# A fused attention, MLP and expert kernel: three blocks of the leading expert instead of two before the slot table

## What is computed

```python
# attention: B, H, S, D = 4, 8, 768, 48
for t in range(S):
    cur = np.einsum('bhd,bhe->bhde', u[None] * kt, vt)
    y[:, :, t] = np.einsum('bhd,bhde->bhe', rt, state + cur)
    state = wt[:, :, :, None] * state + np.einsum('bhd,bhe->bhde', kt, vt)
# MLP on x = y as [3072, 384]; w_in [384, 2048], w_out [2048, 384]
h = x @ w_in
g = np.maximum(h, 0.0) + alpha * np.minimum(h, 0.0)
x = g @ w_out
# top-1 of 8 experts; w1 [8, 384, 1024], w2 [8, 1024, 384]
logits = x @ w_gate
expert_idx = np.argmax(logits, axis=1)
...
for e in range(E):
    mask = expert_idx == e
    ye = np.maximum(x[mask] @ w1[e], 0.0) @ w2[e]
    out[mask] = gate_w[mask, None] * ye
```

## Time and profile before

| | |
|---|---|
| median of 3 runs | 789.07 us (788.85 to 791.1) |
| the profiled execution | 791.64 us, span 789.8 us |
| PE busy | 737.8 us, 93% |
| DVE, ACT, POOL busy | 469.9, 364.5, 391.7 us (59, 46, 50%) |
| mean granted PE clock | 0.979 |
| DMA | 171.61 MB, mean 217 GB/s |
| chain that ended last | PE 66%, DMA 8%, DVE 7%, POOL 5%, issue 5% |

### The profile page before, as it was taken

One profiled execution on the slowest core, in us unless ns is written; L12 is line 12 of the kernel. 1 busy time (PEld: TensorE's weight loads), 2 busy tenths in 40 slices (PEclk: granted clock), 3 DMA queues, 4 the chain that ended last, 5 costly groups with the idle time before them and its releaser, 6 DMA issues.

```text
span 789.8 us, 17773 instructions
## 1 busy us (share of the span) xinstructions
PE 737.8 (93%) x6779; PEld 518.4 (66%) x6779; DVE 469.9 (59%) x959; ACT 364.5 (46%) x734; POOL 391.7 (50%) x372
## 2 busy tenths in 40 slices
PE   4689989989999989999989999997999999999995
PEld 3447655656765666665666666656787878878783
DVE  7995877677768777786786763464433333333331
ACT  3652576647646756646756664462121221212210
POOL 6452567769759759778768875352010101101011
PEclk9987999999999999999999999998999999999998
DMA  8838318372653653645545245797799776776763
GB/s 345 330 131 236 134 62 298 110 250 92 220 213 119 231 211 121 230 140 193 193 151 180 80 160 191 285 419 271 259 394 381 282 246 223 239 263 214 251 232 115
DMA packets 42838, 171.61 MB, mean 217 GB/s; under 512 B 5214, under 2 KB 13152, under 8 KB 37120
## 3 DMA queue, kind: packets, MB, share of 16 engines
q1 hardware_dynamic: 30160, 108.18, 38.8%
q10 hardware_dynamic: 9072, 52.09, 18.7%
q0 software_dynamic: 3520, 10.17, 3.3%
HBM read 133.87 MB, written 37.33 MB: 217 GB/s over the span
## 4 chain that ended last, share of the span: by engine, by line
PE 66%; DMA 8%; DVE 7%; POOL 5%; issue 5%; ACT 3%; SPq 1%; ACTq 1%; POOLq 0%; DVEq 0%
PE bank L1687 5%; PE bank L1689 5%; PE bank L1688 5%; PE bank L1675 5%; PE bank L1676 5%; PE bank L1678 5%; PE bank L1833 4%; PE bank L1831 4%; PE bank L1832 4%; PE bank L1796 4%; PE bank L1797 4%; PE bank L1798 4%; DMA arena<-w_exp_dram 4%; PE bank L1647 2%; DMA route_rows<-xrow,pos 2%
## 5 line engine op out<-in xcount | busy, mean ns | idle before, releaser
L594 POOL TENSOR_TENSOR act_buf<-act_buf 128x384 f16<-128x384 f32 x128 | 119.6, 934 | 148.7 <-ACT act_buf L793 147.8
L1267 DVE SCALAR_TENSOR_TENSOR act_buf<-neg,slope,bank 128x384 f32<-128x384 f32 x128 | 77.8, 608 | 89.4 <-ACT neg L786 88.9
L1687 PE MATMUL bank<-arena,act_buf 128*128 128x392 f16 x384 | 128.2, 334 | 1.5 <-POOL act_buf L594 1.0
L682 POOL DMA_INDIRECT out_dram<-neg,dest x28 | 27.6, 984 | 203.0 <-DVE neg L1520 195.4
L1689 PE MATMUL bank<-arena,act_buf 128*128 128x392 f16 x384 | 128.1, 334 | 0.0
L1688 PE MATMUL bank<-arena,act_buf 128*128 128x392 f16 x384 | 128.1, 334 | 0.0
L1675 PE MATMUL bank<-xh,arena 128*128 128x384 f16 x384 | 126.8, 331 | 1.3 <-DVE act_buf L1267 0.6
L1676 PE MATMUL bank<-xl,arena 128*128 128x384 f16 x384 | 126.7, 331 | 0.0
L1796 PE MATMUL bank<-shared,arena 128*128 128x128 f16 x672 | 116.5, 221 | 1.4 <-DMA arena<-expert_split 1.4
L1797 PE MATMUL bank<-shared,arena 128*128 128x128 f16 x672 | 116.5, 221 | 0.0
L1798 PE MATMUL bank<-shared,arena 128*128 128x128 f16 x672 | 116.4, 221 | 0.0
(11 more groups left out here) (174 smaller groups left out, 1552.3 us busy)
## 6 DMA issues: line engine op xcount, KB each, us to landing
arena<-expert_split ACTq DMA_DIRECT2D x29, 1536.0 KB, 8.2
arena<-w_exp_dram SPq DMA_DIRECT2D x32, 768.0 KB, 7.5
expert_split<-arena SPq DMA_DIRECT2D x32, 768.0 KB, 5.4
arena<-expert_split SPq DMA_DIRECT2D x9, 1536.0 KB, 10.4
arena<-rk_in_dram SPq DMA_DIRECT2D x24, 512.0 KB, 5.5
arena<-rk_tok_dram SPq DMA_DIRECT2D x24, 384.0 KB, 3.6
arena<-w_dram SPq DMA_DIRECT2D x24, 256.0 KB, 6.4
shared<-route_rows ACTq DMA_DIRECT2D x31, 197.0 KB, 2.7
```

The source lines that it names most:

```text
L594: pool.tensor_tensor(gl[:, f % 4, :], gf[:, f % 4, :], gh[:, f % 4, :], ALU.subtract).then_inc(gl_done, 1)
L1687: pe.matmul(at, gh[:, f % 4, ts], woh[:, f, :], start=(f == 0), stop=False)
```

## The change

1. `EARLY = 3`: the leading expert does three blocks ahead of the table. All three use the resident leader weights in `w1_sb[0]` and `w1_sb[1]`. The third need not be full when it is chosen. Its row start is found by a short chain of six DVE steps from the final count (`third_*`), and `third_row_ready` lets ACT load it as soon as all scatters have landed, without the table. The PE order becomes `first(0)`, `first(1)`, `second(0)`, `second(1)` with `turn(2)` inside, `first(2)`, `turn(3)`, `second(2)`, and only then the wait for the table and `step(3)`.
2. The table takes three blocks off the leading expert, at least one is left (`ALU.max` with 1), so there can be one more slot (`SLOTS = 32`).
3. The slots behind take their first weights to `w1_sb[(n - 1) % 3]`; SP's load of expert 0's to `w1_sb[2]` waits for the third block's rows (`x_in[2]`).
4. The second weights of expert 0 are loaded behind half 2's pieces, of expert 1 ahead of half 7's, of experts 2 and 3 between them. Each has a semaphore of its own.
5. Units 50 and 51 get their low parts in half 6 (POOL), the last high of that half moves from f = 14 to 13, and the units of half 7 come at f = 0, 1, 3 to 12 instead of 2 to 13.
6. `load_early_rows` goes from f = 9 to 3, `load_early_w1` from 13 to 12, and `load_early_w2` from behind the last `hidden_high` to f = 15, ahead of `x_high(0)`.

```diff
-SLOTS = TOK // 128 + NE - 1
+SLOTS = TOK // 128 + NE
-EARLY = 2
+EARLY = 3
...
-        HI_AT, HI_AT_START, HI_AT_END = [0, 4, 6, 8, 9, 10, 12, 14], [11, 12, 13, 14], list(range(2, 14))
-        LO_AT, LO_AT_START, LO_AT_END = [4, 5, 7, 8, 9, 10], [12, 13, 14, 15], list(range(2, 14))
+        HI_AT, HI_AT_START, HI_AT_END = [0, 4, 6, 8, 9, 10, 12, 14], [11, 12, 13, 14], [0, 1] + list(range(3, 13))
+        LO_AT, LO_AT_START, LO_AT_END = [4, 5, 7, 8, 9, 10], [12, 13, 14, 15], [0, 1] + list(range(3, 13))
+        HI_AT_SEVENTH, LO_AT_SEVENTH = [0, 4, 6, 8, 9, 10, 12, 13], [4, 5, 7, 8, 9, 10, 13, 14]
...
             for g in range(1, 2 * B - 1):
                 middle(g, FIRST_UNIT[g] // 2)
-            load_w2(0)
+                if g == 2:
+                    sp.wait_ge(wide_free[0], 4)
+                    load_w2(0)
             sp.wait_ge(khat_done, 6 * B)
             sp.wait_ge(qt_done, 6 * B)
             sp.wait_ge(vl_done, 6 * B)
             sp.wait_ge(y_evac, UP + 6 * B)
+            load_w2(1)
             for j in range(FIRST_UNIT[2 * B - 1] // 2, 4 * NE - 1):
                 store_hu(j - 1)
                 load_hu(j + 1)
-                if j % 2 == 0:
-                    load_w2(1 + (j - FIRST_UNIT[2 * B - 1] // 2) // 2)
+                if j in (4 * NE - 5, 4 * NE - 3):
+                    load_w2(2 + (j - (4 * NE - 5)) // 2)
...
-            sp.wait_ge(w1_in[1], 16)
+            sp.wait_ge(x_in[2], 16)
             sp.dma_start(w1_sb[2], wsplit[0][:, 0:2 * UNIT]).then_inc(w1_in[2], 16)
...
-                        if end and f == 9:
+                        if end and f == 3:
                             load_early_rows()
-                        if end and f == 13:
+                        if end and f == 12:
                             load_early_w1()
                         if end and f == 15:
+                            load_early_w2()
                             x_high(0)
...
             hidden_high(2 * B - 1, NF - 1, True)
-            load_early_w2()
             x_high(1)
...
-            for n in range(EARLY):
+            for n in range(2):
                 h_high(n)
-            act.wait_ge(row_tab_ready, 1)
+            act.wait_ge(third_row_ready, 1)
             act.wait_ge(scattered, UPD + 16 * NC * 2 * B)
...
-            for n in range(EARLY, EARLY + 3):
-                load_x(n)
+            load_x(2)
+            act.wait_ge(row_tab_ready, 1)
+            load_x(3)
+            load_x(4)
+            x_high(2)
+            load_x(5)
+            h_high(2)
             act.wait_ge(tab_ready, 1)
-            load_w1(EARLY + 1)
-            x_high(EARLY)
+            load_w1(4)
+            x_high(3)
...
             h_low_part(0, 0)
             dve.wait_ge(rank_evac, 2 * B)
+            dve.scalar_tensor_tensor(out=third_sel[:, :], in0=pick_two[:, :], scalar=1.0 / EARLY, in1=next_row[:, 0:NE],
+                                     op0=ALU.mult, op1=ALU.mult).then_inc(third_chain, 1)
+            dve.wait_ge(third_chain, 1)
+            dve.tensor_reduce(third_row[:, :], third_sel[:, :], AX_X, ALU.add).then_inc(third_chain, 1)
...
+            dve.tensor_copy(slot_tab[0:1, 8:9], third_row[0:1, :]).then_inc(third_row_ready, 1)
...
             h_low_part(1, 1)
             y_out(0)
-            x_low(EARLY)
+            x_low(2)
+            y_out(1)
+            h_low(2)
+            x_low(3)
+            y_out(2)
...
-            for n in range(EARLY):
-                first(n, False)
-            for n in range(EARLY):
-                second(n, None)
+            first(0, False)
+            first(1, False)
+            second(0, None)
+            second(1, None)
+            first(2, False)
+            turn(3)
+            second(2, None)
+            pe.wait_ge(tab_ready, 1)
             for n in range(EARLY, MIN_RUN):
                 step(n)
```

More of the change, by code:

```diff
@@ L313, in build @@
         w1_in = [sem(f"w1_in{i}") for i in range(3)]
-        w2_in = sem("w2_in")
+        w2_in = [sem(f"w2_in{i}") for i in range(NE)]
         x_in = [sem(f"x_in{i}") for i in range(4)]
@@ L475, in middle @@
                     load_tok(b, half, 2)
-            for g in range(1, 2 * B - 1):
-                middle(g, FIRST_UNIT[g] // 2)
             def load_w2(e):
@@ L482, in load_w2 @@
                     sp.wait_ge(split_out[i], UP + 16 * (2 * e + 2))
-                if e > 0:
-                    sp.wait_ge(w2_in, 16 * e)
                 sp.dma_start(arena[:, w2_at(e):w2_at(e) + 2 * UNIT], wsplit[e][:, 2 * UNIT:4 * UNIT]
-                             ).then_inc(w2_in, 16)
-            load_w2(0)
+                             ).then_inc(w2_in[e], 16)
+            for g in range(1, 2 * B - 1):
+                middle(g, FIRST_UNIT[g] // 2)
+                if g == 2:
+                    sp.wait_ge(wide_free[0], 4)
+                    load_w2(0)
             sp.wait_ge(khat_done, 6 * B)
@@ L501, in _ @@
                 sp.wait_ge(split_out[i], UP + 32 * NE)
-            sp.wait_ge(w1_in[1], 16)
+            sp.wait_ge(x_in[2], 16)
             sp.dma_start(w1_sb[2], wsplit[0][:, 0:2 * UNIT]).then_inc(w1_in[2], 16)
-            for i in (2, 3):
-                sp.wait_ge(x_in[i], 16)
+            sp.wait_ge(x_in[3], 16)
             sp.wait_ge(w1_in[0], 32)
@@ L508, in _ @@
             for e in range(4, NE):
+                if e > 4:
+                    sp.wait_ge(w2_in[e - 1], 16)
                 load_w2(e)
@@ L620, in body @@
                         hidden_low(g, f)
-                        if g >= 2 and f == 0:
+                        if g >= 2 and not end and f == 0:
                             unit_low(unit - 2)
-                        if end and f == 1:
-                            unit_low(unit - 1)
                         if start:
@@ L873, in body @@
                     start, end = first and half == 0, last and half == 1
-                    highs = HI_AT_END if end else HI_AT_START if start else HI_AT
+                    highs = HI_AT_END if end else HI_AT_START if start else HI_AT_SEVENTH if g == SEVENTH else HI_AT
                     nb, nh = b + half, 1 - half
@@ L1821, in second @@
                 for f in range(NFE):
-                    if n == EARLY - 1 and f == NFE // 2:
-                        pe.wait_ge(tab_ready, 1)
-                        turn(EARLY)
+                    if n == 1 and f == NFE // 2:
+                        turn(2)
                     fs = slice(f * 128, (f + 1) * 128)
```

47 lines of the change are left out of this document (31 added, 16 removed).

## The result

| | before | after |
|---|---|---|
| median, 20 runs each | 789.14 us (784.65 to 794.83) | 785.54 us (780.0 to 791.83) |
| ratio of the runs | 1 | 0.9945, 95% interval 0.9926 to 0.9964 |
| the profiled execution | 791.64 us | 784.04 us, span 782.3 us |
| PE busy | 737.8 us | 733.9 us |
| mean granted clock | 0.979 | 0.986 |

The kernel became faster by 0.55%: 3.6 us between the medians, 4.3 by the ratio. The profiled executions are 7.6 us apart, more than the change is worth. Half 0, whose code is the same, took 74.97 us in one and 72.09 in the other, since PE's clock fell behind two waits in the first trace (0.50 and 0.66 in the 5 us behind 54.7 and 104.6) and behind the first of them alone in the second (0.66 behind 52.9, 1.00 behind 101.5).

A forecast was written before the change was run, and what follows sets the result against it. PE is busy 93%, so only its waits and slow clock can be won. Of 9.17 us at the change of phase 4.0 return; plus 1.56 in half 7, less 0.4 and 0.6: 5.7 us, giving 783.4 us, range 781.5 to 788.0.

The forecast's parts named there:

- before `second(2)`: Third block: `second(2)` follows `first(2)` with only a turn between, so PE waits 1.1 us for ACT and DVE.
- ACT's place at f = 15: End of half 7: second weights' load ahead of `x_high(0)` in ACT's queue loses 0 to 1.5 us, taken as 0.4.
- After half 7: At `rank(7)`: a wait of 1.08 us instead of 0.71 and 3.77, with no slow clock following.
- DVE becomes late: Middle of `first(1)`: PE waits a new 1.82 us for the low split of (0, 1), behind part of the slot table.
- The last store: End of half 7: last store of splits issued at about 526.7 instead of 533.17, landing 6 to 9.08 us later.
- Second weights of expert 0: Half 3: the 1.5 MB load just before a scatter costs PE between nothing and 3.0 us, taken as 0.6.
- Splits earlier: Halves 6 and 7: two low splits move to half 6, and both waits of half 7 go, 1.56 us won.
- Slots 3 and 4: Weights of slots 3 and 4: no wait, or 4 us at worst for slot 4; the old 1.00 goes.
- Third block: From `first(1)` to `first(3)`: rows arrive in time, so the 1.16 us before `turn(2)` goes; 1.1 comes before `second(2)`.
- A: Change of phase: clock falls all the same behind the waits of 1.08 and 1.82; 785.9 us at worst; chance 0.10.
- B: DMA moves: half 3's scatter costs 3.0 us, or `turn(2)` still waits 1.8, or both (787.6 us); chance 0.22.
- C: ACT's new place for the second weights: if the last store lands late, 1.3 us slower, 790.4 us; chance 0.05.

The follow-up runs named there:

- again: The changed kernel unaltered, profiled and timed a second time beside its variants: 787.28 us, ratio 0.9967 to the kernel before.
- e7: Kernel before with only the phase 1 moves (points 4 to 6), two early blocks and the old slot table: 785.69 us, ratio 0.9943.
- e9: Kernel before with only the new tables of splits, all loads at their old places and two early blocks: 789.31 us, ratio 0.9984.
- e10: Phase 1 moves with two early blocks, but expert 0's second weights mid half 3 and `load_early_w2` back behind the last `hidden_high`: 783.69 us, ratio 0.9914.
- e7_again: Kernel before with only the phase 1 moves and two early blocks, run once more in another group: 784.66 us, ratio 0.9916.
- e6: Changed kernel with the phase 1 moves undone, except `load_early_w2` kept at f = 15: 792.89 us, ratio 1.003.
- e1: Changed kernel with the second weights of expert 0 loaded behind half 6 again: 786.12 us, ratio 0.9951.
- e4: Changed kernel with `load_early_w2` back behind the last `hidden_high`: 786.35 us, ratio 0.996.
- e8: Changed kernel: expert 0's second weights mid half 3, `load_early_w2` back, `h_low_part(0, 1)` before slot table, expert 4's second weights after slot 5's first: 784.37 us, 0.9909.

## Why the prediction was right, and where it wasn't

The time was: 785.5 in 781.5 to 788.0, faster by over 0.3%, 2.1 above the likeliest value.

| step | forecast | trace after | again |
|---|---|---|---|
| old waits and slow clock at the change of phase | -9.17 | gone | gone |
| waits for POOL and DVE in half 7 | -1.56 | gone | gone |
| before `rank(7)` | 1.08 | 1.04 | 1.03 |
| middle of `first(1)` | 1.82 | 1.89 | 1.90 |
| `turn(2)`, slots 3 and 4 | 0 | 0 | 0 |
| before `second(2)` | 1.1 | 1.29 | 1.29 |
| ACT's place at f = 15 | 0.4 | 0.59 | 0.43 |
| half 3 | 0.6 | 1.92 | 1.71 |
| half 7, last scatter | 0 | 0.89 | 0.65 |
| slot 5 | 0 | 1.76 | 0.43 |
| sum | -5.7 | -1.4 | -3.3 |

(The row on ACT's place: 6.85 and 6.69 less 6.26.) The measured 0.9945 and 0.9967 are 4.3 and 2.6 us; the sums are of single traces, and the terms at landings vary from one to the next. The trace after explains 1.4 of the 4.3, and from half 3 on it is only 1.9 shorter than the one before. So 4.3 lies near the forecast's 5.7 partly by luck, since no row shows where the rest comes from.

*After half 7*, *DVE becomes late* and `second(2)` were right to 0.2 us: chains of short instructions, each with a row. The last store took 7.08, inside the 6 to 9.08 assumed, and was issued 4.66 before the last `neg` where the walk had 5.5 (526.7 against 533.72 - 1.56).

*Second weights of expert 0* was mis-sized: 0.6 taken from a range of 0 to 3.0; it measured 1.92 at PE, with nothing covered by DVE (half 3 grew by 1.91). The step that failed is "DVE, full there, would be late too and part of it is covered". The page "DMA: Bandwidth & Descriptors" of the Trainium skill (section "Queues, rings and completion order") says that each engine goes round its queues packet by packet; that the scatter would hardly wait was the prediction's inference from it, and 4.21 against 1.99 does not bear it out.

*Splits earlier* looked only at raw weights. It missed that the same move puts a store and a load of half 7 (484.61 and 485.06) around the last scatter of half 6 (485.61): ACT waits 2.10 for it at 492.47, PE 0.72. *Slots 3 and 4* stopped a slot too soon: the text named slots 4 to 8 as where a lost gain would be, and slot 5 it was.

**The attribution was wrong in part though the sum was near.** *Third block* and *Slots 3 and 4* booked the 1.16 before `turn(2)` and the 1.00 of slot 3 to the third block. e7 shows that the moves alone can remove both, up to 0.57: its last scatter is 5.4 us behind SP's load instead of 2.4. They don't do it in every trace: one of the two waits came back in e9 (2.68 at `turn(2)`), e10 (1.44 there) and e7_again (3.08 at slot 3), and in none of the nine traces with three blocks. I walked the changed program as a whole and never the halves of the change, so I did not see that its headline part brings waits of 2.5 us (1.2 on DVE, 1.3 before `second(2)`) and returns about as much.

*Rivals.* A did not come: the waits of 1.04 and 1.89 lie 6 us apart and the clock is 1.00 in eight windows of 5 us behind `rank(7)`, in nine profiles with the new tables. The Trainium skill ("TensorE: Matmul & The Clock Gate", part 1) ties the rate to how busy the engine has been; that two such waits count together, these traces don't show. B came for half 3, at 1.9 of its 3.0, and not for the third block's rows (scatter issued 543.73, rows loaded at 548.24). C was real, as e6 shows: the walk had `rank(7)` at 549.8, 17.6 after the last `neg`, and e6 has it 17.8 after it. The tables are what disarms it: they bring the last store 3.4 us forward by themselves (e9, issued 3.93 ahead of the last `neg` instead of 0.55), and 4.1 with the loads moved too.

## What to carry to other kernels

Split a change into halves on paper as one does on the chip: walk each part with the others left out, since a wait that three edits remove together may be removed by one of them alone. When one queue both waits for a late store and carries the last work of a stage, move the store, not the wait. And a big load is best placed by asking which small transfer with a waiter is issued within the next few us.

## What the hardware showed

**A scatter is held up by a 1.5 MB load issued just before it.** Time from the last scatter's issue to its landing at the change of phase, by how long SP's load was issued ahead of it: 2.4 ahead (549.11 and 551.50, before) 7.73 us; 3.7 ahead 6.51 (e10); 5.4 and 5.5 ahead 3.93 and 3.98 (e7, e7_again). In the kernel after, where that load is issued behind the scatters, the last one landed 2.75 us after its issue. The chains of waits of e10 and e7:

```profile
546.14 6.51 DMA route_rows<-xrow,pos
```

```profile
550.41 3.93 DMA route_rows<-xrow,pos
```

**The same wait costs the clock in one execution and not in the next.** PE waits 2.14 or 2.15 us for DVE near 288 us in each of the 14 profiles. In the 5 us behind it the clock is 1.00 in seven and about 0.66 in the other seven, some 1.6 us lost; the order of PE's instructions there is the same. The wait comes back every second half: near 163 us the clock falls behind it in eight of the 14, near 412 us in three (e1, e4, e8). What decides it, the runs don't show. This is why half 3 has values 62.0 and 63.7, and 63.9 and 65.4 with the load. Windows of the kernel after, and of its second profile (columns as in the earlier trace rows):

```profile
284.00:289.00 5.00, 2.86 (x19) 1.86 (x19) 4.90 (x12) 2.58 (x5) 2.10 (x3) 1.00 1.01 329
289.00:294.00 5.00, 5.00 (x63) 3.88 (x61) 2.57 (x5) 3.74 (x9) 2.44 (x3) 1.00 0.78 311
```

```profile
289.00:294.00 5.00, 2.86 (x13) 1.46 (x12) 4.90 (x11) 2.58 (x5) 1.91 (x3) 0.80 1.02 383
294.00:299.00 5.00, 5.00 (x58) 3.67 (x57) 2.45 (x6) 3.85 (x9) 2.30 (x3) 0.86 0.70 280
```

From half 7 on, longer waits were followed by a slow stretch in five cases (2.68, 3.08, 3.29, 3.60, 6.34) and not in a sixth (e9's 3.88 at 496.56, 1.00 on both sides). Near 54 us each profile has a wait of 3.15 to 3.17, and the clock falls right behind it in all but e6's. None of the waits up to 1.9 at the change of phase was followed by one. So the price of a wait of 2 us or more is its length plus, in some executions, a slow stretch: 1.6 us in half 3, 2.5 behind `rank(7)` before the change.
